# Windowed attention ahead of a Fourier mix and two MLPs: both heads of a pair in one matmul, with zero blocks, more buffers and a new order

## The reference

```python
for c in range(S // 32):                 # chunks of 32 tokens
    q_c = q[:, :, 32*c : 32*c+32]
    k_full = concat([mem_k, k[l_start:r_end]])   # 8 memory keys, 16 to the left, 32, 8 to the right: 64
    v_full = concat([mem_v, v[l_start:r_end]])
    scores = scale * q_c @ k_full.T
    a = exp(scores - max(scores))
    out[c] = (a / (sum(a) + 1e-9)) @ v_full
x = out, heads side by side: (4, 768, 512)
u = x + real(fft(fft(x, axis=1), axis=2))
x = u + relu(layernorm(u) @ w_ch1) @ w_ch2          # 512 -> 2048 -> 512
h = relu(x @ w_in); y = (h * sigmoid(conv3(h))) @ w_out   # 512 -> 1024 -> 512
```

## Time and profile before

| | |
|---|---|
| median of 3 runs | 1038.44 us (1036.54 to 1039.49) |
| profiled execution, its own time | 1041.72 us |
| its span, first to last instruction | 1039.6 us |
| TensorE busy | 982.4 us, 94% |
| VectorE, ScalarE, GpSimd busy | 43%, 28%, 13% |
| mean granted TensorE clock | 0.975 |
| first `seq` step begins | 44.55 us |
| first `seq` step of the last batch begins | 180.5 us |
| DMA, mean over the span | 92.92 MB, 89 GB/s |

### The profile page before, as it was taken

One profiled execution on the slowest core, in us unless ns is written; L12 is line 12 of the kernel. 1 busy time (PEld: TensorE's weight loads), 2 busy tenths in 40 slices (PEclk: granted clock), 3 DMA queues, 4 the chain that ended last, 5 costly groups with the idle time before them and its releaser, 6 DMA issues.

```text
span 1039.6 us, 18436 instructions
## 1 busy us (share of the span) xinstructions
PE 982.4 (94%) x7896; PEld 884.4 (85%) x7896; DVE 448.6 (43%) x704; ACT 295.7 (28%) x535; POOL 138.5 (13%) x121
## 2 busy tenths in 40 slices
PE   4697877999999999999999999999999999999998
PEld 3586766989999999999999999999998897997996
DVE  3566646645322232222222322224368186294490
ACT  2244534543111111111111111113234243143241
POOL 2534433000000000000000000000014023042041
PEclk8599988999999999999999999999999999999999
DMA  8959665452110200202002002042120110201001
GB/s 309 362 190 349 212 255 185 182 167 97 43 49 1 91 1 1 92 1 88 3 0 91 0 28 63 1 120 94 41 91 1 69 53 24 98 0 40 21 1 61
DMA packets 40644, 92.92 MB, mean 89 GB/s; under 512 B 6144, under 2 KB 6272, under 8 KB 40320
## 3 DMA queue, kind: packets, MB, share of 16 engines
q1 hardware_dynamic: 36544, 82.07, 22.5%
q10 hardware_dynamic: 3456, 6.29, 1.6%
q0 software_dynamic: 576, 3.55, 1.0%
HBM read 66.74 MB, written 25.17 MB: 88 GB/s over the span
## 4 chain that ended last, share of the span: by engine, by line
PE 68%; issue 21%; POOL 6%; DMA 2%; DVE 1%; ACT 1%; ACTq 0%; SPq 0%; POOLq 0%; DVEq 0%
PE ps L809 26%; PE ps L824 26%; PE ps L546 8%; POOL g_lo L1240 6%; PE ps L1184 2%; PE ps L509 2%; PE ps L536 2%; DMA dim_lo<-in_dim_tab 1%; PE ps L520 1%; PE ps L798 1%; PE ps L601 1%; DMA k_win<-in_k 1%; DMA y_scratch<-u_sb 0%; PE ps L1157 0%; ACT mix_sb L379 0%
## 5 line engine op out<-in xcount | busy, mean ns | idle before, releaser
L809 PE MATMUL ps<-un_hi,w 128*128 128x384 f32 x1024 | 285.9, 340 | 1.6 <-ACT mix_sb L387 1.6
L824 PE MATMUL ps<-w,h_hi 128*128 128x512 f32 x768 | 241.1, 395 | 0.0
L809 PEld LDWEIGHTS ps<-un_hi,w 128*128 128x128 f32 x1024 | 187.2, 188 | 6.2 <-ACT mix_sb L387 1.8
L785 DVE SCALAR_TENSOR_TENSOR h_lo<-ps,h_hi 128x384 fp32r<-128x384 f32 x128 | 71.2, 556 | 280.1 <-ACT h_hi L724 280.1
L809 PE MATMUL ps<-un_lo,w 128*128 128x384 f32 x512 | 171.9, 336 | 0.0
L724 ACT ACTIVATE h_hi<-ps 128x384 fp32r<-128x384 f32 x128 | 62.9, 492 | 375.6 <-PE ps L809 375.6
L824 PEld LDWEIGHTS ps<-w,h_hi 128*128 128x128 f32 x768 | 144.0, 188 | 27.5
L824 PE MATMUL ps<-w,h_lo 128*128 128x512 f32 x384 | 149.4, 389 | 0.9 <-DVE h_lo L785 0.9
L1174 PE MATMUL ps<-y_hi,v 128*128 128x384 f32 x512 | 130.7, 334 | 0.8 <-issue 0.8
L1184 PE MATMUL ps<-v,g_hi 128*128 128x512 f32 x384 | 118.8, 391 | 0.0
L1139 DVE SCALAR_TENSOR_TENSOR conv<-h_pad,taps,conv 128x768 f32<-128x768 f32 x64 | 100.5, 1570 | 2.3
(11 more groups left out here) (89 smaller groups left out, 1029.7 us busy)
## 6 DMA issues: line engine op xcount, KB each, us to landing
v_win<-in_v SPq DMA_DIRECT2D x24, 520.0 KB, 7.2
k_win<-in_k SPq DMA_DIRECT2D x24, 512.0 KB, 6.4
w_raw<-in_moe_w SPq DMA_DIRECT2D x16, 512.0 KB, 3.5
q_sb<-in_q SPq DMA_DIRECT2D x24, 256.0 KB, 4.9
x_scratch<-x_sb SPq DMA_DIRECT2D x12, 512.0 KB, 5.2
mix_scratch<-mix_sb ACTq DMA_DIRECT2D x24, 256.0 KB, 5.0
u_sb<-x_scratch SPq DMA_DIRECT2D x8, 768.0 KB, 4.6
mix_in<-mix_scratch SPq DMA_DIRECT2D x8, 768.0 KB, 6.2
```

The lines of the kernel that those rows point to most:

```text
L785: nc.vector.scalar_tensor_tensor(out=h_lo[:, m % 2, :], in0=ps[:, BH + m % 2, 0:HALF], scalar=0.0, in1=h_hi[:, m % 2, :].bitcast(F32), op0 ...
L809: last = nc.tensor.matmul(ps[:, BH + m % 2, 0:HALF], w[:, cols], x[:, par, c, :], start=(k == 0), stop=(k == 3 * ND - 1))
L824: last = nc.tensor.matmul(ps[:, BACC[s], :], h[:, m % 2, cols], w, start=(m == 0 and j == 0), stop=(m == M1T - 1 and j == 2))
```

## The change

A score step takes both heads of a pair in one matmul over all 128 rows of the array. The queries of the two heads lie one above the other as before; the moving keys are a block matrix, k of head u in its 64 partitions and zeros in the other 64, 128 columns wide. The value step does the same with 130 columns. So there are 32 matmuls a step. k_win and v_win get a dimension u and twice the room; their zero blocks are cleared once at the start, keys by VectorE, values by GpSimd, and each load of k or v is issued as two loads of 64 partitions each. All scores of a tile lie in one PSUM bank, and tiles alternate between two banks; a score step waits for the shift of the tile before the last. x_sb becomes two buffers by batch; `norm` waits for fold and store of two batches before. The stores of x stand later in SyncE's queue (n % 6 = 2, 3, 4 behind the q and k loads of that tile). z_lo takes the place of z_raw, so a fold waits for the `seq` steps of the batch before. The table loads increment two semaphores, and `seq0.0` waits for the first two tables, `dim0.0` for the others. k_win moves to the place of the first MLP weights. All four lists of `ORDER` are new; ahead of `seq0.0` now stand eight score, eight turn and six value steps.

```diff
--- before.py
+++ after.py
@@ -97,47 +97,47 @@
 ORDER = {
     "tensor": (
         "scores0.0 scores0.1 turn0.0 values0.0 turn0.1 scores0.2 values0.1 scores0.3 turn0.2 values0.2 "
-        "turn0.3 scores0.4 values0.3 scores0.5 turn0.4 values0.4 scores1.0 turn0.5 values0.5 turn1.0 seq0.0 "
-        "seq0.1 seq0.2 seq0.3 seq0.4 seq0.5 scores1.1 values1.0 dim0.0 turn1.1 scores1.2 seq0.6 values1.1 "
-        "seq0.7 turn1.2 scores1.3 dim0.1 values1.2 scores1.4 turn1.3 values1.3 scores1.5 turn1.4 mix0.0 "
-        "mix0.1 mix0.2 values1.4 mix0.3 scores2.0 mix0.4 turn1.5 mix0.5 values1.5 scores2.1 turn2.0 seq1.0 "
-        "values2.0 seq1.1 turn2.1 seq1.2 scores2.2 seq1.3 values2.1 seq1.4 turn2.2 seq1.5 scores2.3 values2.2 "
-        "dim1.0 scores2.4 turn2.3 seq1.6 values2.3 seq1.7 scores2.5 turn2.4 dim1.1 values2.4 turn2.5 "
-        "scores3.0 mix1.0 mix1.1 mix1.2 values2.5 mix1.3 scores3.1 mix1.4 turn3.0 mix1.5 values3.0 turn3.1 "
-        "scores3.2 seq2.0 values3.1 seq2.1 turn3.2 seq2.2 seq2.3 scores3.3 values3.2 seq2.4 seq2.5 turn3.3 "
-        "scores3.4 values3.3 dim2.0 scores3.5 turn3.4 seq2.6 values3.4 turn3.5 seq2.7 values3.5 dim2.1 mix2.0 "
-        "mix2.1 mix2.2 mix2.3 mix2.4 mix2.5 seq3.0 seq3.1 seq3.2 seq3.3 mlp3 seq3.4 seq3.5 mlp5 dim3.0 mlp7 "
-        "seq3.6 seq3.7 mlp9 dim3.1 mlp10 mix3.0 mix3.1 mix3.2 mix3.3 mlp11 mix3.4 mix3.5 "
+        "turn0.3 scores0.4 values0.3 scores0.5 scores1.0 turn0.4 turn0.5 scores1.1 values0.4 turn1.0 turn1.1 "
+        "values0.5 seq0.0 values1.0 seq0.1 scores1.2 seq0.2 values1.1 seq0.3 turn1.2 seq0.4 values1.2 seq0.5 "
+        "scores1.3 scores1.4 dim0.0 turn1.3 seq0.6 values1.3 seq0.7 turn1.4 scores1.5 scores2.0 dim0.1 "
+        "values1.4 turn1.5 scores2.1 mix0.0 turn2.0 mix0.1 values1.5 mix0.2 scores2.2 mix0.3 values2.0 mix0.4 "
+        "turn2.1 mix0.5 scores2.3 seq1.0 values2.1 seq1.1 scores2.4 seq1.2 turn2.2 seq1.3 turn2.3 seq1.4 "
+        "turn2.4 seq1.5 scores2.5 values2.2 dim1.0 turn2.5 seq1.6 scores3.0 seq1.7 scores3.1 values2.3 dim1.1 "
+        "turn3.0 values2.4 mix1.0 turn3.1 mix1.1 values2.5 mix1.2 scores3.2 mix1.3 values3.0 mix1.4 mix1.5 "
+        "scores3.3 values3.1 seq2.0 seq2.1 turn3.2 seq2.2 scores3.4 seq2.3 turn3.3 seq2.4 scores3.5 seq2.5 "
+        "values3.2 turn3.4 dim2.0 values3.3 seq2.6 turn3.5 seq2.7 values3.4 dim2.1 values3.5 mix2.0 mix2.1 "
+        "mix2.2 mix2.3 mix2.4 mix2.5 seq3.0 seq3.1 seq3.2 seq3.3 seq3.4 mlp3 seq3.5 mlp5 dim3.0 mlp7 seq3.6 "
+        "seq3.7 mlp9 dim3.1 mlp10 mix3.0 mix3.1 mix3.2 mix3.3 mlp11 mix3.4 mix3.5 "
     ),
...
@@ -163,21 +163,25 @@
 
 
     sb.over("span_a")
-    v_win = sb("v_win", [P, NB, 4, HP, D + 1])
-    q_sb = sb("q_sb", [P, NB, HP, P])
+    v_win = sb("v_win", [P, NB, 2, 4, HP, D + 1])
+    x_odd = sb("x_odd", [P, FOLDS, 2, 2, 2, P])
     probs = sb("probs", [P, 2, H, KEYS])
-    stat = sb("stat", [P, 3, 2, 2, HP])
-    sb.over("span_b")
-    k_win = sb("k_win", [P, NB, HP, 4, KEYS])
-    x_sb = sb("x_sb", [P, FOLDS, 2, 2, 2, P])
+    p_sb = sb("p_sb", [P, 2, HP, P])
+    pool_sum = sb("pool_sum", [P, 2, 2, P])
     sb.over("span_c")
-    pool_sum = sb("pool_sum", [P, 2, 2, P])
+    x_even = sb("x_even", [P, FOLDS, 2, 2, 2, P])
     dve_sum = sb("dve_sum", [P, 2, 2, P])
-    p_sb = sb("p_sb", [P, 2, HP, P])
+    top_of = sb("top_of", [P, 2, H])
+    stat = sb("stat", [P, 2, 2, HP, 2])
+    sb.over("w_0")
+    k_win = sb("k_win", [P, NB, 2, HP, 4, KEYS])
+    x_sb = (x_even, x_odd)
     sb.over("w_3")
     z_raw = sb("z_raw", [P, FOLDS, 2, DM])
+    sb.over("z_raw")
+    z_lo = sb("z_lo", [P, FOLDS, 2, DM], F32R)
     z_hi = sb("z_hi", [P, FOLDS, 2, DM], F32R)
-    z_lo = sb("z_lo", [P, FOLDS, 2, DM], F32R)
+    q_sb = sb("q_sb", [P, NB, HP, P])
...
...
@@ -217,14 +223,17 @@
     def bank(step, t, part=0):
         return BF + (PLACE[step][t] + part) % 3
 
-    def by_head(ap):
-        return ap.rearrange("p (a u) k -> p u a k", u=2)
-
-    def fold(eng, api, j, n, sums, added, folded):
+    def zero(api, tile, zeroed):
+
+        for i in range(NB):
+            api.memset(tile[0:P // 2, i, 1], 0.0)
+            api.memset(tile[P // 2:P, i, 0], 0.0).then_inc(zeroed, 1)
+
+    def fold(eng, api, b, j, n, sums, added, folded):
 
 
         group, i = divmod(j, FOLDS)
-        x = x_sb[:, i, :, :, group]
+        x = x_sb[b % 2][:, i, :, :, group]
         api.tensor_tensor(sums[:, 0], x[:, 0], x[:, 1], ALU.add).then_inc(added, 1)
         api.tensor_tensor(sums[:, 1], x[:, 0], x[:, 1], ALU.subtract).then_inc(added, 1)
         eng.wait_ge(added, 2 * n + 2)
@@ -256,26 +265,30 @@
 
                     sp.wait_ge(scored, n - NB + 1)
                 sp.dma_start(q_sb[:, n % NB], q[b, t]).then_inc(ld_qk[n % NB], 16)
-                sp.dma_start(k_win[:, n % NB], k[b, t]).then_inc(ld_qk[n % NB], 16)
+                for u in range(2):
+                    rows = slice(64 * u, 64 * u + 64)
+                    sp.dma_start(k_win[rows, n % NB, u], k[b, t, rows]).then_inc(ld_qk[n % NB], 16)
 
             def load_values(n):
                 b, t = divmod(n, TILES)
                 if n >= NB:
 
                     sp.wait_ge(valued, n - NB + 1)
-                sp.dma_start(v_win[:, n % NB], v[b, t]).then_inc(ld_v[n % NB], 16)
+                for u in range(2):
+                    rows = slice(64 * u, 64 * u + 64)
+                    sp.dma_start(v_win[rows, n % NB, u], v[b, t, rows]).then_inc(ld_v[n % NB], 16)
 
             def store_x(b, i):
                 sp.wait_ge(x_ready, b * TILES + FOLDS + i + 1)
-                sp.dma_start(x_dram[b, :, i].rearrange("e p (a g r) -> p e a g r", a=2, g=2), x_sb[:, i]).then_inc(st_x[i], 16)
+                sp.dma_start(x_dram[b, :, i].rearrange("e p (a g r) -> p e a g r", a=2, g=2), x_sb[b % 2][:, i]).then_inc(st_x[i], 16)
 
 
             for n in range(B * TILES):
                 load_tile(n)
+                if n > TILES and n % TILES in STORED:
+                    store_x((n - 2) // TILES - 1, (n - 2) % TILES)
                 if n > 0:
                     load_values(n - 1)
-                if n >= TILES and n % TILES < FOLDS:
-                    store_x(n // TILES - 1, n % TILES)
             load_values(B * TILES - 1)
             for i in range(FOLDS):
@@ -286,20 +299,20 @@
             def load_tables():
 
                 pool.wait_ge(scored, 5)
-                for dst, src in ((seq_hi, seq_tab[0]), (seq_lo, seq_tab[1]), (dim_hi, dim_tab[0]), (dim_lo, dim_tab[1])):
-                    pool.dma_start(dst[:], src).then_inc(ld_tab, 16)
+                for dst, src, landed in ((seq_hi, seq_tab[0], ld_seq), (seq_lo, seq_tab[1], ld_seq),
+                                         (dim_hi, dim_tab[0], ld_dim), (dim_lo, dim_tab[1], ld_dim)):
+                    pool.dma_start(dst[:], src).then_inc(landed, 16)
 
             def folds(b, j):
                 n = 4 * b + ON_POOL.index(j)
                 pool.wait_ge(x_ready, b * TILES + j + 1)
                 if b > 0:
 
-                    pool.wait_ge(pool_lo_ready, n - 3)
-                    pool.wait_ge(z_hi_ready, (b - 1) * TILES + j + 1)
+                    pool.wait_ge(seq_done, 8 * (b - 1) + 4 * (j // FOLDS + 1))
                 if n > 0:
 
                     pool.wait_ge(pool_folded, n)
-                fold(pool, nc.gpsimd, j, n, pool_sum, pool_added, pool_folded)
+                fold(pool, nc.gpsimd, b, j, n, pool_sum, pool_added, pool_folded)
 
             def lower(b, j):
@@ -310,6 +323,8 @@
                 nc.gpsimd.tensor_tensor(of_unit(z_lo, j), of_unit(z_raw, j), of_unit(z_hi, j).bitcast(F32), ALU.subtract
                                         ).then_inc(pool_lo_ready, 1)
 
+            zero(nc.gpsimd, v_win, v_zeroed)
+            pool.wait_ge(v_zeroed, NB)
             for step, b, t in steps_of("gpsimd"):
                 if step == "fold":
                     folds(b, t)
@@ -417,40 +432,40 @@
             def shift(b, t):
                 n = b * TILES + t
                 dve.wait_ge(scored, n + 1)
-                s4 = ps[:, BS:BS + 2, 0:HP * KEYS].rearrange("p u (a k) -> p u a k", a=HP)
-                top = stat[:, 0, t % 2]
-                nc.vector.tensor_reduce(top, s4, AX, ALU.max).then_inc(max_done, 1)
+                rows = ps[:, BS[t % 2], :].rearrange("p (h k) -> p h k", h=H)
+                top = top_of[:, t % 2]
+                nc.vector.tensor_reduce(top, rows, AX, ALU.max).then_inc(max_done, 1)
                 dve.wait_ge(max_done, n + 1)
                 if n >= 2:
 
                     dve.wait_ge(p_turned, n - 1)
-                nc.vector.tensor_tensor(by_head(probs[:, t % 2]), s4, top.unsqueeze(3).to_broadcast([P, 2, HP, KEYS]),
-                                        ALU.subtract).then_inc(shift_done, 1)
+                nc.vector.tensor_tensor(probs[:, t % 2], rows, top.unsqueeze(2).to_broadcast([P, H, KEYS]), ALU.subtract
+                                        ).then_inc(shift_done, 1)
 
             def normalise(b, t):
```

(59 more changed lines are left out.)

9 lines of the change are left out of this document (6 added, 3 removed), and 42 rows, old and new, of the table ORDER.

## The result

The changed kernel takes 1054.81 us (median of 6 runs, 1051.35 to 1058.51) against 1037.72 (median of 6, 1036.54 to 1040.56): a ratio of 1.0161, 95% interval 1.0134 to 1.0189. It is 17 us slower, where I had forecast 12 faster; the time lies above the range.

The account below looks back on a forecast made before the run. TensorE is busy 94% of the span; the idle time and reduced clock that matter lie before 180.5 us. Terms -3.5 + 6.8 - 10 - 5 - 1 = -12.7 us against 1038.4 gave 1026 us, range 1016 to 1048.

Parts of the forecast that it names:

- the cost of the loads: Ahead of seq0.0: five loads a tile in place of three, 0.43 us each, under the 3.3 us of a tile's bytes.
- The rival: k and v loads to 64 partitions run at half rate: +6.3 us in total, 1045 (1038 to 1052); chance 0.25.
- the estimate of +4 us: k and v loads, by the skill's figures, take 1.67 times their time: +4 of the half-rate case's +6.3 us.
- the order: Ahead of seq0.0: one score and one turn more, yet seq0.0 at 41 us (38 to 44.5), -3.5 us.
- SyncE's queue would run ahead: Ahead of seq0.0: later stores of x and a second x buffer let the queue run ahead; part of the -3.5 us.
- The array time: Score and value steps between seq0.0 and seq3.0: 0.87 us each at full clock, 0.99 with the switch; +6.8 us.
- the rival at 1061: Score and value steps: weight loads are not hidden, +35 us less 13; chance 0.05, shared with 4 cycles a column.
- The fetch stalls: TensorE's idle time put down to issue behind seq0.0, 17.8 us: fewer instructions take off 10 us.
- The rival that they stay (1041): Late fetches come from what stands in the DMA queues, so the terms of 10 and 5 go: +2.3 us; chance 0.12.
- The clock from seq0.0 to seq3.0: Half-clock stretches behind three issue gaps run at full clock: -5 us, clock of that stretch 0.95 or more.
- m_all: TensorE's 3.1 us wait for m_all: a value step moved behind dim2.1 fills 1 us of it, -1 us.
- The zeros and the folds: Clearing zero blocks (at most 8.3 and 16 us) lies inside the spread; folds, some 9 us, are hidden behind other work.

Follow-up runs that it names:

- all_ports: The changed kernel with the two heads of a pair interleaved on even and odd partitions, so each load spreads over all 128 partitions: 1033.39 us, ratio 0.9958.
- moved: all_ports with two places changed in VectorE's list (lower0.2 behind shift0.5, bl3.0 ahead of mlp0): 1030.90 us, ratio 0.9927.
- double_count: all_ports with each score and value matmul cut into two, 64 a step with the same array work: 1047.37 us, ratio 1.0082.
- split_rows: The kernel before with each k and v load issued as two loads of 64 partitions: 1061.51 us, ratio 1.0243.
- split_cols: The kernel before with each k and v load issued as two loads of 128 partitions, half of each row: 1036.65 us, ratio 0.9993.
- three_loads: The kernel before with three 6.3 MB load blocks put ahead: 128 partitions, halves of 64, every second partition; 1104.77 us in one execution.

## Why the prediction was wrong, step by step

**The step that failed is the cost of the loads, taken as nothing but issue time** ("2.15 us in all, under the 3.3 us that the bytes of a tile take"), with 396 GB/s for the lead-in. In halves the rate is 0.56 of the full one, and that costs 21.4 us (all_ports against after). The rival had the mechanism and nearly the price: 19.0 us (14 + 5), deciding below 0.6. That price was for half the rate. At the 0.56 measured, the same terms give 14.1 - 4 + 3.9 = 14.0 us, so its nearness is in part luck, and its total of 1045 was passed by 10 us as well. I gave it half the forecast's chance, arguing that drifting engines would serve both halves at once. The block in halves put 24 loads into one queue, where such a drift could have come, and the rate stayed at 229 GB/s: the weight was wrong. By the figures of the Trainium skill that the prediction cites (SBUF — State Buffer, "Door 1: The DMA port swizzle") the rate would have been 0.60 of full, against 0.56 measured; that deserved more than my guess. But the estimate of +4 us that I made of them does not come out of the terms: 1.67 times the time adds 12 - 4 + 3.3 = 11.3 us, which makes -1.4.

**The second is the order, which was costed as one more score and turn ahead of seq0.0 and nothing else.** With fast loads seq0.0 came at 45.0, not 41, and at 38.9 in the old order; of the 4.0 us missed 1.2 lie in a place that moved recovered. I had added the term up from TensorE's work at half clock, 33 us. In all_ports TensorE was busy for 25.2 us of that time, at a clock of 0.96, and idle for 19.9, so the waits for keys, shifts and exponentials set it and not the array. The last batch's Fourier steps took 39.5 us, not 34.8; no term was there for it. With slow loads the eighth score step waited for keys that landed 10.3 us behind those of the seventh; I had priced its bytes at 396 GB/s. I had also said that SyncE's queue would run ahead. Its stores do wait less (12.8 us in place of 54.3), but its v loads wait 72.8 us for value steps in place of 22.9.

**Right were these.** The array time: with 32 matmuls a step, two score steps at full clock begin 1.88 us ahead of the next step, 0.87 each with 0.12 for the switch, as worked out from the earlier trace rows (PE's timeline of after):

```profile
88.58 1.95 PE L527 MATMUL ps<-k_win,q_sb 128*32 128x128 f32 x64
90.46 0.44 PE L565 MATMUL ps<-b_hi,dim_lo 128*128 128x386 f32 x1
```

Weight loads stay hidden in these 0.87 us with all row groups shared, and the rival at 1061 had no part in the loss. By the rule of the Trainium skill cited in the prediction (TensorE: Matmul & The Clock Gate, Part 3, "The mechanism") each group would add a load; the trace doesn't show one.

The fetch stalls: I took 10 of 17.8 us, and all went, with the 10.2 ahead of 60 us too; double_count shows that the number of instructions makes them. The rival that they stay (1041) falls, though its condition has a part: in split_rows they grew with slower transfers alone. The clock from seq0.0 to seq3.0 is 0.96, as forecast, and 0.97 in all_ports. TensorE's busy time there is 113.2 us before and after, where +6.8 and -5 would make 115.0. What that clock is worth for the whole kernel is open: two executions of the kernel before, at mean clocks of 0.977 and 0.990, took 1036.7 us each. m_all: 3.1 to 0.8 us, 2.3 gained where 1 was forecast. The zeros and the folds cost nothing that a wait shows. The middle then took 129.1 us where 126.8 was forecast, and 123.1 without the slow loads. That it came near is two misses that offset each other, stalls priced too low and slow loads not priced. And it took 131.5 us in split_cols, which is as fast as the kernel before, so part of the gain against 135.95 is one execution against another.

**Made anew** from the same terms, with the measured sizes: lead-in +0.5, middle -12.9 and end +4.7 are all_ports, -7.7 by the spans; slow loads add 16.0, 6.0 and -1.5. Together +12.8, the difference of the spans; the 4.3 us up to the difference of the medians lie in the profiled execution of the kernel before.

## What to carry to other kernels

When an edit cuts a load by partitions, price it by the partitions that each piece fills, not by its bytes: a layout that interleaves what has to be kept apart (even and odd partitions) gave the same block matrices at 0.90 of the full rate in three_loads. Where many small matmuls run beside full DMA queues, count the instructions as well as the columns: gaps of "issue" in the middle of a block went with their number and grew when the loads beside them slowed down; half the instructions for the same array work was worth 14.0 us. An order written for fast transfers has to be timed again when they slow down; look for the load that lands last ahead of the first step that needs them all. The longest wait of the queue was not the one that cost: the transfers ahead of it kept the DMA engines busy.
